# Queries' high parts made by POOL, and the keys' rotation put behind both parts of the queries

## The chip, the cores and the metric

The kernel runs on one core of one Trainium2 chip. The metric is the device time of one execution in microseconds (us). The core's engines run side by side, each with its own list of instructions that it executes in order: TensorE (PE, matmuls), VectorE (DVE), ScalarE (ACT), GpSimd (POOL), and SyncE (SP), which here issues DMA transfers. They meet only at semaphores: an instruction waits until a counter has reached a value that others raise.

## The reference

Rotary attention over 2 batches, 8 heads, 576 tokens and 64 elements per head, then two dense blocks of 512 to 2048 to 512 over all 1152 tokens, the first gated by a sigmoid, the second with an ELU. All in 32-bit floats. Cut to what matters:

```python
def rotate(x):
    x1, x2 = (x[..., :half], x[..., half:])
    return np.concatenate([x1 * cos - x2 * sin, x1 * sin + x2 * cos], axis=-1)
q_rot, k_rot = (rotate(q), rotate(k))
scores = scale * np.matmul(q_rot, k_rot.transpose(0, 1, 3, 2))
scores = scores - np.max(scores, axis=-1, keepdims=True)
attn = np.exp(scores)
attn = attn / (np.sum(attn, axis=-1, keepdims=True) + 1e-09)
x = np.matmul(attn, v)                        # then tokens x 512
h = x @ w_in; x = (h * (1.0 / (1.0 + np.exp(-h)))) @ w_out
h = x @ w_in2; y = np.where(h > 0.0, h, np.exp(np.minimum(h, 0.0)) - 1.0) @ w_out2
```

## The kernel before, in words

**Split numbers.** PE multiplies a rounded 32-bit format (float32r). To keep precision every operand is split into a high part (a copy rounded to float32r) and a low part (the value less its high part), and a product is the sum of three matmuls (high by low, high by high, low by high). So each operand costs a cast and a subtraction on ACT, DVE or POOL.

**Tiles and stages.** The 1152 tokens are three chunks of 384. A chunk has 8 heads, which makes 24 head steps i, each with 3 tiles of 128 queries against 576 keys. A tile goes: scores on PE (L822, L824), negated row maximum on DVE (L620), exponential on ACT (L449), transposes on PE (L838, L847), high part on ACT (L457), low part on DVE (L627). After a head's three tiles come the products with the values (L868, L870) and the steps that scale the output and split it for the dense layers (L475, L651, L657, L482, L662). The dense layers of a chunk are 64 units of weights, 128 x 512 each (L903), each loaded by SP, cast by ACT (L489) and subtracted by POOL (L331). The first chunk's attention runs alone, up to about 65 us (the first stage); the attention of chunks 2 and 3 is spread between the dense units of the chunk before.

**Preparation of queries and keys.** Heads come in pairs, one on partitions 0 to 63 and one on 64 to 127. For pair r the raw queries (`q_raw`, 2 x 384 columns, two buffers) and keys (`k_raw`, 2 x 576 columns, two buffers; only pairs 0 to 7) are loaded. POOL rotates them: two products with the cosine and sine table (L303; keys L286) and their sum (L308; keys L291). ACT casts the high part into the second half of the same buffer (`queries_hi` L434; `keys_hi` L430). POOL subtracts for the low part (`queries_lo` L313; `keys_lo` L296). SP then copies both parts to where PE reads them (`place`, L217 to L223), and after that the buffer is free for the load of pair r + 2. Values are cast by ACT (`values_hi`, L440) and subtracted by POOL (`values_lo`, L318).

**What sets the order.** Nothing is scheduled by a program: each engine's list is written out by hand in loops. In the first stage POOL does, per pair: rotate queries, rotate keys, queries' low part, one weight cast (from the third pair on, L323), keys' low part, values' low part. ACT walks the 24 tiles with `exp_tile(n)` and `probs_hi(n - 1)`, and puts the preparation between them: in the even head of a pair `queries_hi` behind tile 0, `keys_hi` behind tile 1, `values_hi` behind tile 2. Later, in the dense loop, the same steps stand at fixed units j of a head's eight: for example `queries_hi` on ACT at j == 3 of the odd head and `queries_lo` on POOL at j == 5. The queries of pair 5 are rotated just ahead of the dense loop, with their cast on ACT at n == 1.

Of the kernel before, what the change touches and what calls it, by code (L numbers as in the profile page):

```python
# [15 lines left out]
F32R = mybir.dt.float32r  # L16
# [27 lines left out]
def build(nc, q, k, v, rope, w, out):  # L44
    with ExitStack() as ctx:
# [234 lines left out]
        def _(pool):  # L280
# [24 lines left out]
            def queries_add(r):  # L305
                raw = q_raw[r % 2]
                pool.wait_ge(q_scaled, 2 * r)
                nc.gpsimd.tensor_tensor(raw[:, 0, :], raw[:, 0, :], raw[:, 1, :], ALU.add).then_inc(q_roped, 1)  # L308

            def queries_lo(r):  # L310
                raw = q_raw[r % 2]
                pool.wait_ge(q_hi_done, r)
                nc.gpsimd.tensor_tensor(raw[:, 0, :].bitcast(F32R), raw[:, 0, :], raw[:, 1, :], ALU.subtract) \  # L313
                    .then_inc(q_lo_done, 1)
# [33 lines left out]
            def rope_queries(r):  # L348
                queries_times(r, 0)
                queries_times(r, 1)  # L350
                queries_add(r)

            def rope_keys(r):
                keys_times(r, 0)
                keys_times(r, 1)
                keys_add(r)

            rope_queries(1)
            rope_keys(1)
            queries_lo(1)  # L360
            keys_lo(1)
            values_lo(0)
            for p in range(1, 4):
                rope_queries(p + 1)
                rope_keys(p + 1)
                queries_lo(p + 1)
                if p > 1:
                    first_weight_hi(p - 2)
                keys_lo(p + 1)
                values_lo(p)  # L370
            first_weight_hi(2)
            for n in range(AHEAD):
                weight_lo(n)
            rope_queries(5)
            rope_keys(5)
            for n in range(ALL_UNITS):
                i, j = H + n // 8, n % 8
                p = i // 2
                r = p + 2
                if n + AHEAD < ALL_UNITS:  # L380
                    weight_lo(n + AHEAD)
                if n < 2:
                    pool.wait_ge(scored, QN * (7 + n))
                    nc.gpsimd.memset(q_one[n][:, PADS].bitcast(F32), 0.0).then_inc(pads_zero, 1)
                    nc.gpsimd.memset(q_two[n][:, PADS].bitcast(F32), 0.0).then_inc(pads_zero, 1)
                if n == 2:
                    queries_lo(5)
                    keys_lo(5)
                if i % 2 == 0:
                    if j == 5 and p < 8:  # L390
                        values_lo(p)
                    if r < 8:
                        if j == 3:
                            keys_times(r, 0)
                        if j == 4:
                            keys_times(r, 1)
                        if j == 6:
                            keys_add(r)
                    if r < ITERS // 2 and j == 7:
                        queries_times(r, 0)  # L400
                else:
                    if r < ITERS // 2:
                        if j == 0:
                            queries_times(r, 1)
                        if j == 1:
                            queries_add(r)
                    if r < 8 and j == 3:
                        keys_lo(r)
                    if r < ITERS // 2 and j == 5:
                        queries_lo(r)  # L410

# [3 lines left out]
        def _(act):  # L415
# [12 lines left out]
            def keys_hi(r):  # L428
                act.wait_ge(k_roped, r)
                nc.scalar.copy(k_raw[r % 2][:, 1, :].bitcast(F32R), k_raw[r % 2][:, 0, :]).then_inc(k_hi_done, 1)  # L430

            def queries_hi(r):
                act.wait_ge(q_roped, r)
                nc.scalar.copy(q_raw[r % 2][:, 1, :].bitcast(F32R), q_raw[r % 2][:, 0, :]).then_inc(q_hi_done, 1)  # L434

            def values_hi(r):
                act.wait_ge(v_in, 16 * (r + 1))
# [104 lines left out]
            for n in range(H * QN):  # L542
                i, t = n // QN, n % QN
                p = i // 2
                exp_tile(n)
                if n:
                    probs_hi(n - 1)
                if t == 0 and i:
                    end_hi(i - 1)
                if t == 0 and i >= 2:  # L550
                    copy_out_lo(i - 2)
                if i % 2 == 0:
                    if t == 0:
                        queries_hi(p + 1)
                    if t == 1:
                        keys_hi(p + 1)
                    if t == 2:
                        values_hi(p)
                elif p:
                    if t == 0:  # L560
                        widen_sums(p - 1)
                    if t == 2:
                        output_hi(p - 1)
# [3 lines left out]
            for n in range(ALL_UNITS):  # L567
# [21 lines left out]
                    output_hi(p - 1)  # L589
                if not beside:  # L590
                    continue
                if n in (1, 2):
                    (queries_hi if n == 1 else keys_hi)(5)
                if j == 2 and not first:
                    copy_out_lo(i - 1)
                if i % H == H - 1 and j == 7:
# [10 lines left out]
                else:  # L607
                    if j == 0 and p + 2 < 8:
                        keys_hi(p + 2)
                    if j == 3 and p + 2 < ITERS // 2:  # L610
                        queries_hi(p + 2)
            evict_a(ALL_UNITS - 1)


# [436 lines left out]
```

## Time and profile before

| | |
|---|---|
| time, median of 3 runs | 568.55 us (568.23 to 568.56) |
| profiled execution | 568.11 us, its span 566.3 us |
| PE busy | 537.8 us, 95% of the span |
| ACT busy | 349.3 us, 62% |
| POOL busy | 346.8 us, 61% |
| DVE busy | 287.1 us, 51% |

An engine's busy share is a mean over stages that have different limits. The chain that ended last is followed back from the last instruction, at each step to whatever released it; the share of an engine in it says how much of the time that engine's work was what the rest waited for. A timeline row gives the start, the duration, the engine, the line and the tiles, and in brackets how long the engine had been idle before and what ended that. Instructions of one engine can overlap by a few hundredths of a microsecond.

### The profile page before, as it was taken

What the parts mean: (1) busy time and instruction counts of PE and PEld (TensorE: products, weight loads), DVE (VectorE), ACT (ScalarE), POOL (GpSimd) and SP (SyncE); (2) the same over time, 40 slices, a digit from 0 to 9 for tenths busy, and PEclk for the clock granted to TensorE, in tenths of its full rate; (3) what the DMA queues carried; (4) which work ended last, traced back from release to release, by engine and by line L of the source; (5) the groups of instructions that cost most, each with busy time, mean ns of one, the idle gap of its engine ahead of it and who ended that gap; (6) DMA issues with size and microseconds to landing.
All of it is one profiled execution on the core that took longest, in us unless ns stands there. A gap on an engine that the chain in (4) does not pass through costs nothing.

```text
span 566.3 us, 9272 instructions
## 1 busy us (share of the span) xinstructions
PE 537.8 (95%) x3308; PEld 526.8 (93%) x3308; DVE 287.1 (51%) x503; ACT 349.3 (62%) x726; POOL 346.8 (61%) x287
## 2 busy tenths in 40 slices
PE   1888899999999999999999999999999999999997
PEld 1777889999999999999999999989999999999997
DVE  5788766633267763246663336775334540057500
ACT  3899678755467665557785456666555763356531
POOL 5999989669636556555654653444545666655662
PEclk9999999999999999999999999999999999999999
DMA  8676726456355345344333433324433444433440
GB/s 323 186 233 189 218 82 175 114 188 165 97 152 142 90 132 162 106 129 154 116 121 119 128 113 84 105 94 134 120 106 110 132 132 126 131 112 113 131 157 29
DMA packets 43229, 77.16 MB, mean 136 GB/s; under 512 B 5296, under 2 KB 12848, under 8 KB 43184
## 3 DMA queue, kind: packets, MB, share of 16 engines
q1 hardware_dynamic: 41456, 74.21, 44.4%
q10 hardware_dynamic: 1728, 2.36, 1.1%
q8 instruction: 27, 0.44, 0.3%
q14 instruction: 18, 0.15, 0.1%
HBM read 63.57 MB, written 2.36 MB: 116 GB/s over the span
## 4 chain that ended last, share of the span: by engine, by line
PE 79%; DVE 10%; ACT 6%; issue 3%; DMA 1%; SPq 0%; ACTq 0%; DVEq 0%
PE banks L903 61%; PE banks L868 5%; PE banks L838 5%; PE banks L822 3%; PE banks L824 3%; DVE banks L692 2%; DVE act_buf L690 2%; ACT prob L449 2%; DVE neg_max L620 2%; ACT act_buf L501 1%; PE banks L847 1%; DVE pt_lo L627 1%; DMA k_raw<-k 1%; DVE g_lo L698 1%; ACT g_hi L508 1%
## 5 line engine op out<-in xcount | busy, mean ns | idle before, releaser
L331 POOL TENSOR_TENSOR w_lo<-w_raw,w_hi 128x512 fp32r<-128x512 f32 x192 | 247.0, 1288 | 201.4 <-ACT w_hi L489 201.0
L489 ACT CAST w_hi<-w_raw 128x512 fp32r<-128x512 f32 x189 | 117.1, 621 | 40.3 <-PE banks L903 36.1
L903 PE MATMUL banks<-x_lo,w_hi 128*128 128x384 f32 x384 | 130.7, 340 | 1.5 <-DVE g_lo L698 0.8
L903 PE MATMUL banks<-g_lo,w_hi 128*128 128x384 f32 x384 | 129.1, 336 | 0.0
L903 PE MATMUL banks<-x_hi,w_lo 128*128 128x384 f32 x384 | 128.7, 335 | 0.0
L903 PE MATMUL banks<-x_hi,w_hi 128*128 128x384 f32 x384 | 128.6, 335 | 0.0
L903 PE MATMUL banks<-g_hi,w_lo 128*128 128x384 f32 x384 | 128.5, 335 | 0.0
L903 PE MATMUL banks<-g_hi,w_hi 128*128 128x384 f32 x384 | 128.5, 335 | 0.0
L627 DVE TENSOR_TENSOR pt_lo<-banks,pt_hi 128x512 fp32r<-128x512 f32 x60 | 41.3, 688 | 93.5 <-ACT pt_hi L457 93.4
L449 ACT ACTIVATE prob<-banks,neg_max 128x576 f32<-128x576 f32 x72 | 53.6, 744 | 42.5 <-DVE neg_max L620 42.2
L903 PEld LDWEIGHTS banks<-x_lo,w_hi 128*128 128x128 f32 x384 | 72.1, 188 | 5.0 <-DVE x_lo L662 1.6
L698 DVE SCALAR_TENSOR_TENSOR g_lo<-banks,g_hi 128x384 fp32r<-128x384 f32 x96 | 53.4, 556 | 40.5 <-ACT g_hi L508 40.2
L903 PEld LDWEIGHTS banks<-g_lo,w_hi 128*128 128x128 f32 x384 | 72.1, 188 | 0.1
L903 PEld LDWEIGHTS banks<-x_hi,w_hi 128*128 128x128 f32 x384 | 72.2, 188 | 0.0
L903 PEld LDWEIGHTS banks<-g_hi,w_hi 128*128 128x128 f32 x384 | 72.2, 188 | 0.0
L903 PEld LDWEIGHTS banks<-g_hi,w_lo 128*128 128x128 f32 x384 | 72.1, 188 | 0.0
L903 PEld LDWEIGHTS banks<-x_hi,w_lo 128*128 128x128 f32 x384 | 72.1, 188 | 0.0
L508 ACT ACTIVATE g_hi<-banks 128x384 fp32r<-128x384 f32 x96 | 47.4, 493 | 35.6 <-DVE banks L692 30.6
L822 PE MATMUL banks<-k_st,q_one 128*128 128x288 f32 x160 | 51.8, 340 | 11.5 <-DVE q_two L676 11.4
L501 ACT ACTIVATE act_buf<-banks 128x384 f32<-128x384 f32 x96 | 46.9, 489 | 21.1 <-PE banks L903 21.0
L620 DVE TENSOR_REDUCE neg_max<-banks 128x1 f32<-128x576 f32 x72 | 54.0, 750 | 6.6 <-PE banks L824 6.0
L838 PE MATMUL banks<-ident,prob 128*128 128x128 f32 x288 | 44.9, 279 | 10.9 <-ACT prob L449 10.5
(75 smaller groups left out, 696.0 us busy)
## 6 DMA issues: line engine op xcount, KB each, us to landing
w_raw<-w SPq DMA_DIRECT2D x192, 256.0 KB, 2.7
q_raw<-q SPq DMA_DIRECT2D x11, 384.0 KB, 3.5
q_one<-q_raw SPq DMA_DIRECT2D x44, 96.0 KB, 2.5
k_raw<-k SPq DMA_DIRECT2D x7, 576.0 KB, 4.5
k_st<-k_raw SPq DMA_DIRECT2D x28, 144.0 KB, 2.5
v_raw<-v SPq DMA_DIRECT2D x8, 320.0 KB, 3.1
out<-act_buf ACTq DMA_DIRECT2D x12, 192.0 KB, 2.7
q_two<-q_raw SPq DMA_DIRECT2D x22, 96.0 KB, 2.3
```

Source lines behind the costliest of these rows:

```text
L331: nc.gpsimd.tensor_tensor(w_st[LO][:, slot, :], w_raw[:, slot, :], w_st[HI][:, slot, :].bitcast(F32), ALU.subtract).then_inc(w_lo_done, 1)
L449: nc.scalar.activation(halves(prob[:, n % 3, :]), scores(n), ACT.Exp, bias=neg_max[:, n % 2:n % 2 + 1], accum_out=row_sum[:, i // 2 % 2, t ...
L489: nc.scalar.copy(w_st[HI][:, slot, :], w_raw[:, slot, :]).then_inc(w_hi_done, 1)
L501: nc.scalar.activation(act_buf[:, ft % 2, :], mlp(USES * c + 20 * layer + ft), func, scale=scale) \
L508: nc.scalar.activation(g[HI][:, ft, :], mlp(USES * c + 20 * layer + ft), ACT.Copy, scale=(0.5, 1.0)[layer]).then_inc(g_hi_done, 1)
L620: nc.vector.tensor_reduce(neg_max[:, n % 2:n % 2 + 1], scores(n), AXES.XY, ALU.max, negate=True) \
L627: nc.vector.tensor_tensor(pt[LO][buffer_of(i)][:, :, tokens], probs_t(n), pt[HI][buffer_of(i)][:, :, tokens].bitcast(F32), ALU.subtract) \
L698: nc.vector.scalar_tensor_tensor(g[LO][:, ft, :], mlp(USES * c + 20 * layer + ft), (0.5, 1.0)[layer], g[HI][:, ft, :].bitcast(F32), ALU.mu ...
L822: nc.tensor.matmul(scores(n)[:, a, :], q_one[par][:, col:col + P], k_st[:, slot, keys], start=m == 0, stop=False)
L838: last = nc.tensor.transpose(probs_t(n)[:, m, :], prob[:, n % 3, m * P:(m + 1) * P], ident[:, :])
L868: nc.tensor.matmul(pv_out[:, cols], v_st[:, slot, m, :], pt[part][buf][:, m, cols], start=m == 0 and part == LO, stop=False)
L903: last = nc.tensor.matmul(dst, w_st[wp][:, slot, m * P:(m + 1) * P], src[xp][:, tile, :], start=start and n == 0, stop=stop and n == 2)
```

## The change

POOL gets a function `queries_hi`, which copies the queries' sum, rounded, into the second half of the buffer, and ACT loses its function of that name with its 11 calls. In the first stage POOL's order per pair becomes: rotate queries, high part, low part, then rotate keys, and so on; for pair 5 the high part stands ahead of the keys' rotation and the low part stays where it was; for later pairs the high part is made at j == 4 of the odd head. Nothing else differs. (Line numbers behind the edit move: L313 of the new kernel is the new cast, and its `queries_lo` is L318.)

```diff
--- before.py
+++ after.py
@@ -307,6 +307,11 @@
                 pool.wait_ge(q_scaled, 2 * r)
                 nc.gpsimd.tensor_tensor(raw[:, 0, :], raw[:, 0, :], raw[:, 1, :], ALU.add).then_inc(q_roped, 1)
 
+            def queries_hi(r):
+                raw = q_raw[r % 2]
+                pool.wait_ge(q_roped, r)
+                nc.gpsimd.tensor_copy(raw[:, 1, :].bitcast(F32R), raw[:, 0, :]).then_inc(q_hi_done, 1)
+
             def queries_lo(r):
                 raw = q_raw[r % 2]
                 pool.wait_ge(q_hi_done, r)
@@ -356,14 +361,16 @@
                 keys_add(r)
 
             rope_queries(1)
+            queries_hi(1)
+            queries_lo(1)
             rope_keys(1)
-            queries_lo(1)
             keys_lo(1)
             values_lo(0)
             for p in range(1, 4):
                 rope_queries(p + 1)
+                queries_hi(p + 1)
+                queries_lo(p + 1)
                 rope_keys(p + 1)
-                queries_lo(p + 1)
                 if p > 1:
                     first_weight_hi(p - 2)
                 keys_lo(p + 1)
@@ -372,6 +379,7 @@
             for n in range(AHEAD):
                 weight_lo(n)
             rope_queries(5)
+            queries_hi(5)
             rope_keys(5)
             for n in range(ALL_UNITS):
                 i, j = H + n // 8, n % 8
@@ -406,6 +414,8 @@
                             queries_add(r)
                     if r < 8 and j == 3:
                         keys_lo(r)
+                    if r < ITERS // 2 and j == 4:
+                        queries_hi(r)
                     if r < ITERS // 2 and j == 5:
                         queries_lo(r)
 
@@ -428,10 +438,6 @@
             def keys_hi(r):
                 act.wait_ge(k_roped, r)
                 nc.scalar.copy(k_raw[r % 2][:, 1, :].bitcast(F32R), k_raw[r % 2][:, 0, :]).then_inc(k_hi_done, 1)
-
-            def queries_hi(r):
-                act.wait_ge(q_roped, r)
-                nc.scalar.copy(q_raw[r % 2][:, 1, :].bitcast(F32R), q_raw[r % 2][:, 0, :]).then_inc(q_hi_done, 1)
 
             def values_hi(r):
                 act.wait_ge(v_in, 16 * (r + 1))
@@ -550,8 +556,6 @@
                 if t == 0 and i >= 2:
                     copy_out_lo(i - 2)
                 if i % 2 == 0:
-                    if t == 0:
-                        queries_hi(p + 1)
                     if t == 1:
                         keys_hi(p + 1)
                     if t == 2:
@@ -589,8 +593,8 @@
                     output_hi(p - 1)
                 if not beside:
                     continue
-                if n in (1, 2):
-                    (queries_hi if n == 1 else keys_hi)(5)
+                if n == 2:
+                    keys_hi(5)
                 if j == 2 and not first:
                     copy_out_lo(i - 1)
                 if i % H == H - 1 and j == 7:
@@ -607,8 +611,6 @@
                 else:
                     if j == 0 and p + 2 < 8:
                         keys_hi(p + 2)
-                    if j == 3 and p + 2 < ITERS // 2:
-                        queries_hi(p + 2)
             evict_a(ALL_UNITS - 1)
```

POOL's list in the first stage, one pair (the one whose queries are rotated from 20.78 us on). Before; `q_raw` and `k_raw` are the raw and rotated queries and keys, `v_st` the values, and in brackets stand the semaphores waited for:

```order
L303 TENSOR_TENSOR q_raw<-q_raw,table 128x384 [waits q_in0]
L303 TENSOR_TENSOR q_raw<-q_raw,table 128x384
L308 TENSOR_TENSOR q_raw<-q_raw 128x384 [waits q_scaled]
L286 TENSOR_TENSOR k_raw<-k_raw,k_table 128x576 [waits k_table_in,k_in0]
L286 TENSOR_TENSOR k_raw<-k_raw,k_table 128x576
L291 TENSOR_TENSOR k_raw<-k_raw 128x576 [waits k_scaled]
L313 TENSOR_TENSOR q_raw<-q_raw 128x384 [waits q_hi_done]
L296 TENSOR_TENSOR k_raw<-k_raw 128x576 [waits k_hi_done]
L318 TENSOR_TENSOR v_st<-v_raw,v_st 128x2x5x64 [waits v_hi_done]
```

The same pair in the changed kernel:

```order
L303 TENSOR_TENSOR q_raw<-q_raw,table 128x384 [waits q_in0]
L303 TENSOR_TENSOR q_raw<-q_raw,table 128x384
L308 TENSOR_TENSOR q_raw<-q_raw 128x384 [waits q_scaled]
L313 CAST q_raw<-q_raw 128x384 [waits q_roped]
L318 TENSOR_TENSOR q_raw<-q_raw 128x384 [waits q_hi_done]
L286 TENSOR_TENSOR k_raw<-k_raw,k_table 128x576 [waits k_table_in,k_in0]
L286 TENSOR_TENSOR k_raw<-k_raw,k_table 128x576
L291 TENSOR_TENSOR k_raw<-k_raw 128x576 [waits k_scaled]
L296 TENSOR_TENSOR k_raw<-k_raw 128x576 [waits k_hi_done]
L323 TENSOR_TENSOR v_st<-v_raw,v_st 128x2x5x64 [waits v_hi_done]
```

The sum of the keys (L291) stood behind five instructions of its pair and stands behind seven; between it and the keys' low part (L296), which waits for ACT's cast of the keys, stood the queries' low part, and now nothing does.

ACT's list for the same pair, before; `prob` is an exponential's tile, `pt_hi` the transposed one's high part:

```order
L475 COPY head_out<-banks 64x384 [waits pv_done]
L434 CAST q_raw<-q_raw 128x384 [waits q_roped]
L449 ACTIVATE prob,row_sum<-banks,neg_max 128x576 [waits end_transposed,max_done]
L457 CAST pt_hi<-banks 128x4x128 [waits pv_done,transposed]
L430 CAST k_raw<-k_raw 128x576 [waits k_roped]
L449 ACTIVATE prob,row_sum<-banks,neg_max 128x576 [waits end_transposed,max_done]
L457 CAST pt_hi<-banks 128x4x128 [waits transposed]
L440 CAST v_st<-v_raw 128x2x5x64 [waits v_in]
```

And in the changed kernel:

```order
L481 COPY head_out<-banks 64x384 [waits pv_done]
L455 ACTIVATE prob,row_sum<-banks,neg_max 128x576 [waits end_transposed,max_done]
L463 CAST pt_hi<-banks 128x4x128 [waits pv_done,transposed]
L440 CAST k_raw<-k_raw 128x576 [waits k_roped]
L455 ACTIVATE prob,row_sum<-banks,neg_max 128x576 [waits end_transposed,max_done]
L463 CAST pt_hi<-banks 128x4x128 [waits transposed]
L446 CAST v_st<-v_raw 128x2x5x64 [waits v_in]
```

The cast of `q_raw` is gone; the cast of `k_raw`, which waits for the keys' sum (`k_roped`), stands where it stood, with the same instructions behind it.

## Rows read from the trace of the kernel before

**Rows 1.** from the page: busy us by engine, and the chain by engine

```profile
PE 537.8 (95%) x3308; PEld 526.8 (93%) x3308; DVE 287.1 (51%) x503; ACT 349.3 (62%) x726; POOL 346.8 (61%) x287
...
PE 79%; DVE 10%; ACT 6%; issue 3%; DMA 1%; SPq 0%; ACTq 0%; DVEq 0%
```

**Rows 2.** windows: stretch, length, busy us (instructions) by engine, PEclk, DMA share, GB/s

```profile
14.00:62.00 48.00, 39.18 (x269) 36.30 (x270) 40.29 (x68) 43.87 (x99) 44.37 (x38) 1.00 0.70 194
82.00:92.00 10.00, 10.00 (x62) 9.96 (x61) 7.52 (x14) 8.55 (x19) 10.00 (x9) 1.00 0.52 153
```

**Rows 3.** timeline of ACT: start, duration, instruction, idle before

```profile
16.55 0.67 ACT L430 CAST k_raw<-k_raw 128x576 fp32r<-128x576 f32 x1 [0.45 <-POOL k_raw L291]
...
28.45 0.68 ACT L430 CAST k_raw<-k_raw 128x576 fp32r<-128x576 f32 x1
...
30.21 0.75 ACT L440 CAST v_st<-v_raw 128x640 fp32r<-128x640 f32 x1
...
41.48 0.68 ACT L430 CAST k_raw<-k_raw 128x576 fp32r<-128x576 f32 x1
...
54.52 0.68 ACT L430 CAST k_raw<-k_raw 128x576 fp32r<-128x576 f32 x1
...
61.56 0.74 ACT L449 ACTIVATE prob<-banks,neg_max 128x576 f32<-128x576 f32 x1 [0.54 <-DVE neg_max L620]
...
74.61 0.51 ACT L434 CAST q_raw<-q_raw 128x384 fp32r<-128x384 f32 x1
```

**Rows 4.** timeline of POOL, 9 to 63 us

```profile
9.25 1.95 POOL L303 TENSOR_TENSOR q_raw<-q_raw,table 128x384 f32<-128x384 f32 x2 [0.50 <-DVE banks L730]
...
15.10 1.41 POOL L291 TENSOR_TENSOR k_raw<-k_raw 128x576 f32<-128x576 f32 x1
...
19.27 1.54 POOL L318 TENSOR_TENSOR v_st<-v_raw,v_st 128x640 fp32r<-128x640 f32 x1 [0.43 <-ACT v_st L440]
20.78 1.96 POOL L303 TENSOR_TENSOR q_raw<-q_raw,table 128x384 f32<-128x384 f32 x2
22.81 1.01 POOL L308 TENSOR_TENSOR q_raw<-q_raw 128x384 f32<-128x384 f32 x1
23.78 2.81 POOL L286 TENSOR_TENSOR k_raw<-k_raw,k_table 128x576 f32<-128x576 f32 x2
26.67 1.41 POOL L291 TENSOR_TENSOR k_raw<-k_raw 128x576 f32<-128x576 f32 x1
...
32.55 1.96 POOL L303 TENSOR_TENSOR q_raw<-q_raw,table 128x384 f32<-128x384 f32 x2
...
45.59 1.96 POOL L303 TENSOR_TENSOR q_raw<-q_raw,table 128x384 f32<-128x384 f32 x2
...
51.47 1.63 POOL L291 TENSOR_TENSOR k_raw<-k_raw 128x576 f32<-128x576 f32 x1
...
59.18 3.74 POOL L331 TENSOR_TENSOR w_lo<-w_raw,w_hi 128x512 fp32r<-128x512 f32 x3
```

**Rows 5.** groups by form, POOL: count, busy us, mean ns, idle before

```profile
L313 POOL TENSOR_TENSOR q_raw<-q_raw 128x384 fp32r<-128x384 f32 x11 | 11.1, 1008 | 0.5 <-ACT q_raw L434 0.5
...
L323 POOL CAST w_hi<-w_raw 128x512 fp32r<-128x512 f32 x3 | 1.8, 612 | 0.0
```

**Rows 6.** timeline of PE, waits at the end of the stage

```profile
60.60 0.33 PE L838 MATMUL banks<-ident,prob 128*128 128x128 f32 x1 [1.37 <-ACT prob L449]
...
64.73 0.34 PE L903 MATMUL banks<-x_lo,w_hi 128*128 128x384 f32 x1
...
72.27 0.44 PE L903 MATMUL banks<-x_lo,w_hi 128*128 128x384 f32 x1 [0.74 <-DVE x_lo L662]
...
80.36 0.66 PE L838 MATMUL banks<-ident,prob 128*128 128x128 f32 x4 [0.51 <-ACT prob L449]
```

**Rows 7.** timeline of PE, matmuls of 288 columns

```profile
17.33 0.44 PE L824 MATMUL banks<-k_st,q_two 128*128 128x288 f32 x1
...
18.93 0.29 PE L822 MATMUL banks<-k_st,q_one 128*128 128x288 f32 x1
```

## The prediction

> **What bounds the kernel now.** I read the page's chain first [rows 1]: TensorE (PE) carries 79% of it, ScalarE (ACT) 6% and VectorE (DVE) 10%, and POOL none of its listed lines. So the changed instructions are not on the bound by themselves, and the question is where they gate something. The windows [rows 2] split the program into two regimes. In 82 to 92 us, inside the dense layers, PE is busy 10.00 of 10.00 us; what another engine does there is hidden as long as its slots suffice. In 14 to 62 us, the attention of the first eight heads, no engine is full, but ACT (43.87 of 48 us) and POOL (44.37 of 48 us) come close and PE does not (39.18). That stage is set by engines handing work to each other, and the order of instructions on ACT and POOL is what counts. It works in four pairs of heads (I number them 1 to 4; the pair's preparation is for the next heads).
>
> The timeline of ACT [rows 3] has, in each pair, the cast of the queries' high parts (L434, 0.51 us as the one at 74.61, which stands in the dense layer), then an exponential, a copy, and the cast of the keys' high parts (L430). L430 needs the keys' sum from POOL (L291). POOL's timeline [rows 4] gives when that sum is there. Pair 1: sum ends 15.10 + 1.41 = 16.51, L430 starts 16.55 after a wait of 0.45. Pair 2: 26.67 + 1.41 = 28.08 against 28.45, slack 0.37. Pair 4: 51.47 + 1.63 = 53.10 against 54.52, slack 1.42. Pair 3 repeats pair 4 to 0.01 us, 13.04 us earlier (L430 at 41.48), so its sum ends 40.06. That slack is the number the change works on.
>
> **What is removed.** ACT loses 11 casts of 0.51 us. Four stand in the first stage, one (74.61) [rows 3] early in the first dense layer, six later, where PE is full.
>
> **What is added and moved on POOL.** In each of the four pairs the keys' rotation now stands behind two instructions more: the high cast and the low subtraction. The trace has no 384-element cast on POOL; the nearest row is its 512-element cast at 0.612 us [rows 5]. Bounds: 0.46 us (scaled by elements) and 0.61 us (none of it scales). I take 0.50, near the scaled end, because the subtractions show a small fixed part: 1.008 us for 384 elements [rows 5], 1.25 us from start to start for 512 (59.18, three in 3.74) [rows 4]. The sum of the queries starts 22.81 and lasts 1.01; before, the keys started at 23.78. Now: 22.81 + 1.01 + 0.07 (the gap that POOL shows before an instruction that waits for its predecessor, 20.78 + 1.96 to 22.81) + 0.50 + 0.07 + 0.96 (the subtraction of 1.008 less the 0.05 that consecutive starts overlap) = 25.42, so **1.64 us later** per pair; by the bounds 1.60 to 1.75.
>
> The Trainium skill (GPSIMD Engine Reference, section 3.1) gives as best case of a tight one-input loop 1.8 cycles per element, 769 ns for 512 elements. This trace has 612 ns for 512, so the measurement decides; by the page the 384-element cast would be an estimated 576 ns and the sum below 0.3 us longer.
>
> **What that meets.** ACT executes in order. Behind the waiting L430 stand the next exponential, the copy of the transposed tile and the cast of the values (L440), for which POOL's last step of the pair (L318) waits. So POOL and ACT form a loop: pair start S, keys' sum end, 0.04, ACT's run from L430 to the end of L440 (28.45 to 30.21 + 0.75 = 2.51), 0.07, values' low part 1.51 start to start (19.27 to 20.78), next S. The old low subtraction and the weight cast used to stand between sum and keys' low part; that cover goes, and POOL idles while ACT casts the keys. Walking it:
> - Pair 1: S = 9.25. Sum end 16.51 + 1.64 = 18.15, L430 at 18.19 (was 16.55), next S = 18.19 + 4.09 = 22.28 (was 20.78).
> - Pair 2: before, S to sum end took 28.08 - 20.78 = 7.30; now 8.94. L430 at 31.26 (was 28.45), next S 35.35 (was 32.55).
> - Pair 3: 7.51 as in pair 4, now 9.15. L430 at 35.35 + 9.15 + 0.04 = 44.54 (was 41.48), next S 48.63 (was 45.59).
> - Pair 4: 53.10 - 45.59 = 7.51, now 9.15. L430 at 57.82 (was 54.52): **+3.30 us**.
>
> So the first two pairs lose 1.6 and 1.2 and the others 0.25 each, since there POOL had been waiting for ACT and the 0.51 us that ACT saves just turns into a longer wait at L430. Does ACT really arrive early? It reaches L430 of pair 4 no later than 54.52 + 3.06 (the lateness in pair 3) - 0.51 = 57.1, before 57.82. Yes, and likewise in pair 3.
>
> **What is given back.** After the last L430 ACT runs without a gap until the exponential at 61.56, which waited 0.54 for a maximum of DVE [rows 3]. PE and DVE have run on during ACT's hold, so I take 0.46 of that back: the dense layer, whose first matmul stood at 64.73 [rows 6], starts 2.84 later. POOL must have the first three weights' low parts by then: they began 59.18 and took 3.74 [rows 4], now 3.3 later, ending 66.2 against 67.6: covered, though the margin shrinks from 1.8 to 1.4. In 70 to 82 us the chain passes L434 at 74.61; without it the activation behind it starts some 0.4 earlier, and the PE wait of 0.51 at 80.36 [rows 6] shrinks by that much. After that PE is full and nothing is regained; the six POOL casts of the later pairs (6 x 0.50) lie in POOL's idle time (it is busy 61% of the span [rows 1]), and ACT's six saved casts lie beside PE. On SP the query placements of each pair now start earlier, the key placements later by the same shift as ACT; I count nothing for them.
>
> Sum: 3.30 - 0.46 - 0.40 = +2.44 us. The profiled execution took 568.11 (span 566.3 and 1.8 around it), so it would take 570.55; the median of the runs is 568.55, 0.44 above it, so I predict **571.0 us**. With the bounds of the cast (-0.04 x 4, +0.11 x 4), 0 to 0.54 given back at the exponential and 0 to 0.5 at L434, the likeliest case spans 570.7 to 572.3.
>
> **Rivals.**
> 1. *The slack absorbs it.* The most the tail can give back is what PE waited there: 1.37 at 60.60, 0.74 at 72.27, 0.51 at 80.36 [rows 6], together 2.62. Then 3.30 - 2.62 = +0.7, about 569.25. For it: DVE and PE had finished their part during the hold. Against: the first and second of these waits are for ACT's and DVE's steps that themselves shift. Chance 0.14.
> 2. *Faster: ACT's relief wins.* If the keys' sum still came before ACT asked for it, five casts of 0.51 on the chain would go: 2.5 us, 566.0. It decides only if the delay on POOL stays below the slack of the pair: 1.64 against 0, 0.37 and twice 1.42. That holds only if most of the inserted 1.5 us runs under something. For it: L434 is on the chain of waits in pairs 2 to 4 and is surely removed. Against: POOL shows no idle place before the sum. Chance 0.08.
> 3. *The array's clock.* The page's granted clock is 1.00 throughout, yet the matmuls of 288 columns take 0.44 us at 17.33 and 0.29 at 18.93 [rows 7], the pace of the 1.2 and of the 2.4 GHz level, so PE came up near 18 us after steady work. A hold of ACT would leave PE idle some 1.6 us per pair, more than the 1.37 us at 60.60, after which the dense matmul at 64.73 still took 0.34 us. If the clock fell in pairs 2 to 4: a pair holds 39.18 x 13.04 / 48 = 10.6 us of PE [rows 2], 0.44 / 0.29 = 1.5 times as long at the slow pace, thus 5.3 us more; for half of the pair 2.7, less some 0.9 by which ACT is early at the next hold: 3 x 1.8 = 5.4, about 576.4. Chance 0.06. The Trainium skill (TensorE: Matmul & The Clock Gate, section "HAM oscillation") says that pauses between bursts can bring the slow clock back each time; this trace shows no fall after the pause of 1.37 us.
>
> **How the numbers follow.** Forecast 0.72, rivals 0.14, 0.08 and 0.06. A measurement of this kernel tells about 0.2%, 1.1 us, from no change. Slower by more than that: 0.72 + 0.06 = 0.78; within: 0.14; faster: 0.08. Range for 8 in 10: from 569.4, near the first rival, to 572.5, just over the likeliest case's end.
>
> **What would show it.** In the new profile: the 11 L434 casts gone from ACT and 11 POOL casts of about 0.50; keys' high casts at about 18.2, 31.3, 44.5 and 57.8 with waits of 1 to 2 us on POOL's sum; POOL waiting about 0.7 for them; the first dense matmul near 67.6; from 85 us on the same work shifted by about 2.4. It is wrong if ACT does not wait at the keys' cast, if the POOL cast takes well under 0.4 us, or if PE's wait near 82 vanishes with more than 0.5.

## The result, and the profile after

| | before | after |
|---|---|---|
| time, median of 6 runs | 568.55 us (568.17 to 568.70) | 572.46 us (571.21 to 572.77) |
| ratio | | 1.0066 (95% interval 1.0053 to 1.0079) |
| profiled execution | 568.11 us, span 566.3 | 572.77 us, span 570.7 |

The change makes the kernel slower by 0.66%, 3.9 us between the medians. That is forecast in sign and inside the range, but 1.5 us above the predicted 571.0.

From the page after: PE's share of the busy time, the granted clock in 40 slices, and the chain by engine, which now has POOL in it [rows 1].

```profile
PE 541.9 (95%) x3308; PEld 530.5 (93%) x3308; DVE 288.6 (51%) x503; ACT 345.1 (60%) x715; POOL 352.6 (62%) x298
...
PEclk9989999999999999999999999999999999999999
...
PE 78%; DVE 9%; ACT 6%; issue 4%; POOL 2%; DMA 1%; SPq 0%; ACTq 0%; DVEq 0%; POOLq 0%
```

POOL's timeline after, first pair (start, duration, instruction, idle before). The cast takes 0.50 us; the sum of the keys starts at 16.75 instead of 15.10 [rows 4], and then POOL idles 0.78 us for ACT's cast of the keys.

```profile
12.36 0.50 POOL L313 CAST q_raw<-q_raw 128x384 fp32r<-128x384 f32 x1
12.94 1.00 POOL L318 TENSOR_TENSOR q_raw<-q_raw 128x384 fp32r<-128x384 f32 x1
13.90 2.77 POOL L286 TENSOR_TENSOR k_raw<-k_raw,k_table 128x576 f32<-128x576 f32 x2
16.75 1.42 POOL L291 TENSOR_TENSOR k_raw<-k_raw 128x576 f32<-128x576 f32 x1
18.95 1.41 POOL L296 TENSOR_TENSOR k_raw<-k_raw 128x576 fp32r<-128x576 f32 x1 [0.78 <-ACT k_raw L440]
```

ACT's timeline after: the four casts of the keys (L430 before, L440 now). Three wait for POOL's sum, the third does not.

```profile
18.20 0.67 ACT L440 CAST k_raw<-k_raw 128x576 fp32r<-128x576 f32 x1 [2.09 <-POOL k_raw L291]
...
31.29 0.67 ACT L440 CAST k_raw<-k_raw 128x576 fp32r<-128x576 f32 x1 [1.12 <-POOL k_raw L291]
...
45.18 0.68 ACT L440 CAST k_raw<-k_raw 128x576 fp32r<-128x576 f32 x1
...
59.21 0.67 ACT L440 CAST k_raw<-k_raw 128x576 fp32r<-128x576 f32 x1 [0.70 <-POOL k_raw L291]
```

Before, they stood at 16.55, 28.45, 41.48 and 54.52 [rows 3]. The first two are where the prediction put them (18.19, 31.26). The last two are late by 0.6 and 1.4 us more, and PE's timeline shows where most of that comes from (experiment 1 gives its size): after an idle of 1.55 us its matmuls of 288 columns take 0.44 us, the pace of the 1.2 GHz level [rows 7], until about 41 us.

```profile
37.33 1.00 PE L840 MATMUL banks<-ident,prob 128*128 128x128 f32 x4 [1.55 <-ACT prob L455]
...
38.36 0.44 PE L826 MATMUL banks<-k_st,q_two 128*128 128x288 f32 x1
...
41.09 0.29 PE L826 MATMUL banks<-k_st,q_two 128*128 128x288 f32 x1
```

The windows after give the granted clock there (the column behind POOL's): 0.94, then 0.64. The kernel before has 1.00 in both.

```profile
34.00:38.00 4.00, 1.91 (x14) 1.63 (x13) 3.51 (x6) 3.93 (x10) 3.92 (x4) 0.94 0.56 135
38.00:42.00 4.00, 4.00 (x23) 3.98 (x22) 2.09 (x4) 1.92 (x5) 3.86 (x5) 0.64 0.76 193
```

### The profile page after: what moved, and what is told of

It reads as the page before. It is cut to its first block, busy times and chain, and to the rows that moved or that the text cites. A ratio compares the mean times of both kernels' runs of the same rounds, so it can differ in the third digit from the quotient of the medians.

```text
span 570.7 us, 9272 instructions
## 1 busy us (share of the span) xinstructions
PE 541.9 (95%) x3308; PEld 530.5 (93%) x3308; DVE 288.6 (51%) x503; ACT 345.1 (60%) x715; POOL 352.6 (62%) x298
## 4 chain that ended last, share of the span: by engine, by line
PE 78%; DVE 9%; ACT 6%; issue 4%; POOL 2%; DMA 1%; SPq 0%; ACTq 0%; DVEq 0%; POOLq 0%
PE banks L905 62%; PE banks L870 4%; PE banks L840 4%; PE banks L824 3%; PE banks L826 3%; DVE banks L694 2%; ACT prob L455 2%; DVE act_buf L692 2%; DVE neg_max L622 2%; ACT act_buf L507 1%; PE banks L849 1%; DMA k_raw<-k 1%; DVE pt_lo L629 1%; ACT g_hi L514 1%; PE banks L883 1%
## 5 line engine op out<-in xcount | busy, mean ns | idle before, releaser
L336 POOL TENSOR_TENSOR w_lo<-w_raw,w_hi 128x512 fp32r<-128x512 f32 x192 | 247.4, 1290 | 197.6 <-ACT w_hi L495 197.2
L824 PE MATMUL banks<-k_st,q_one 128*128 128x288 f32 x160 | 53.1, 347 | 11.4 <-DVE q_two L678 11.4
L840 PE MATMUL banks<-ident,prob 128*128 128x128 f32 x288 | 46.7, 287 | 11.1 <-ACT prob L455 10.9
```

The costliest lines, as they stand in the source:

```text
L336: nc.gpsimd.tensor_tensor(w_st[LO][:, slot, :], w_raw[:, slot, :], w_st[HI][:, slot, :].bitcast(F32), ALU.subtract).then_inc(w_lo_done, 1)
L824: nc.tensor.matmul(scores(n)[:, a, :], q_one[par][:, col:col + P], k_st[:, slot, keys], start=m == 0, stop=False)
L840: last = nc.tensor.transpose(probs_t(n)[:, m, :], prob[:, n % 3, m * P:(m + 1) * P], ident[:, :])
```

## The experiments

Each kernel was timed against the kernel before on the same chip; the medians of before there were 568.20 to 568.27.

**1. The changed kernel again** (no edit).

> The changed kernel once more, unaltered, for a second profile and more times. The first profile showed matmuls of 288 columns at 0.44 us between 37 and 40 us and a granted clock of 0.87 there; two of its six runs took 571.2 to 571.5 at a mean clock of 0.999, four took 572.4 to 572.8 at 0.997. Theory A (the keys' late sum holds ACT, and the clock adds a part of its own): the runs fall in these two groups again, 571.3 with a mean clock of 0.999 and 572.5 with 0.997, and the base of the loss is the lower one. Theory B (the clock's fall is only a symptom): times do not sort by the mean clock.

Measured: 571.68 us median of 5 runs (571.53 to 573.15), ratio 1.0066 (1.0054 to 1.0078). Over the 11 runs of both series, five took 571.2 to 571.7 (median 571.5) at mean clocks of 0.997 to 1.0, six took 572.4 to 573.2 (median 572.6) at 0.994 to 0.997. So there are two groups, 1.1 us apart, but the mean clock does not sort them strictly: the profiled execution, 571.59 us, has 0.997. Its windows show where its slow stretch lies, which is ahead of 26 us:

```profile
18.00:22.00 4.00, 2.27 (x15) 1.76 (x15) 2.37 (x4) 3.61 (x8) 2.79 (x3) 0.96 0.37 89
22.00:26.00 4.00, 4.00 (x23) 3.85 (x22) 3.22 (x5) 3.19 (x8) 3.86 (x5) 0.61 0.44 102
```

It cost nothing there, because POOL sets the pace: the first two casts of the keys stand 13.10 us apart, against 31.29 - 18.20 = 13.09 in the first profile, where the clock was 1.00 in that stretch. Where the clock falls matters, not only whether. In the first profile it fell in 34 to 42 us, and from POOL's first step to ACT's fourth cast of the keys that execution takes 59.21 - 9.26 = 49.95 us, this one 58.26 - 9.47 = 48.79: 1.16 more, the distance between the groups. This trace is the clean case, and I use it for the balance below. ACT's casts of the keys in it, each waiting for POOL:

```profile
18.39 0.67 ACT L440 CAST k_raw<-k_raw 128x576 fp32r<-128x576 f32 x1 [2.08 <-POOL k_raw L291]
...
31.49 0.67 ACT L440 CAST k_raw<-k_raw 128x576 fp32r<-128x576 f32 x1 [1.30 <-POOL k_raw L291]
...
44.88 0.67 ACT L440 CAST k_raw<-k_raw 128x576 fp32r<-128x576 f32 x1 [0.69 <-POOL k_raw L291]
...
58.26 0.68 ACT L440 CAST k_raw<-k_raw 128x576 fp32r<-128x576 f32 x1 [0.69 <-POOL k_raw L291]
```

**2. The low part back behind the keys** (in the changed kernel).

```diff
             queries_hi(1)
-            queries_lo(1)
             rope_keys(1)
+            queries_lo(1)
```

(and the same in the loop over the pairs)

> POOL keeps the cast right behind the queries' sum, but the low part goes back behind the keys' rotation in the first stage. The keys' sum is then late by 0.57 us per pair instead of 1.64. Theory A (what costs is how late the keys' sum is when ACT asks for it): S to sum 7.83, 7.87, 8.08, 8.08; keys' casts at about 17.1, 29.1, 41.5 and 54.0; 568.0 (567.4 to 568.8), no slower than the kernel before. Theory B (the 0.5 us more of POOL's work per pair is what costs, wherever it stands): about the same as the changed kernel, 571 to 572.

Measured: 569.54 us (569.34 to 570.84), ratio 1.0028 (1.0017 to 1.0039). Two thirds of the loss go with this move, though POOL does the same work: place decides, not amount. It stays 1.3 us above before, where I expected none. The casts of the keys are at 17.28, 29.26, 42.54 and 55.52. The first two wait for the sum (1.00 and 0.42 us) and stand near the expected 17.1 and 29.1. The last two, expected at 41.5 and 54.0, wait for nothing: there ACT itself is late, behind a wait of 1.26 us at 38.35 for DVE's scaled output, and PE had before that waited 0.46 us for a placement of the keys at 36.41. So the sum's lateness is not the whole of this kernel's loss. It also carries the collision of experiments 7 and 8 (DVE's step takes 1.03 us here).

**3. Both parts behind the keys** (in the changed kernel).

```diff
-            queries_hi(1)
-            queries_lo(1)
             rope_keys(1)
+            queries_hi(1)
+            queries_lo(1)
```

> In the first stage POOL makes the queries' high and low parts behind the keys' rotation, so that they cover ACT's cast of the keys. The keys' sum is not late at all within the pair, ACT keeps its 0.51 us per pair. Theory A: no wait of ACT at the keys' casts in pairs 2 to 4, POOL's period is 11.8 to 12.6 us against ACT's 12.5; the dense layer starts 1.0 to 1.4 us earlier than in the kernel before; 567.0 (566.3 to 567.8), faster than before. Theory B (POOL's work itself costs): 570 to 572.

Measured: 568.86 us (567.51 to 570.71, 12 runs), ratio 1.0010 (0.9999 to 1.0021): no change, and a spread of 3 us. The loss of the change is gone with POOL's extra work still in place, but the gain that I expected did not come. The casts of the keys are at 16.79, 28.86, 41.91 and 54.58, unhindered; but POOL ends the pair later, the placements follow, and PE now waits for one:

```profile
23.51 0.37 PE L824 MATMUL banks<-k_st,q_one 128*128 128x288 f32 x1 [0.74 <-DMA k_st<-k_raw]
```

Six of the twelve runs lie at 567.5 to 568.4 and six at 569.3 to 570.7. Four of the slower six have a mean clock of 1.0, so the clock does not make this split; its cause stays open.

**4. One more cast on POOL in each pair of the changed kernel.**

```diff
                 pool.wait_ge(q_roped, r)
+                if r < 5:
+                    nc.gpsimd.tensor_copy(spare[:, :], raw[:, 0, 0:352])
                 nc.gpsimd.tensor_copy(raw[:, 1, :].bitcast(F32R), raw[:, 0, :]).then_inc(q_hi_done, 1)
```

> The changed kernel, with one more cast of 352 columns into an unused tile ahead of the queries' cast for pairs 1 to 4 (its result is not used). It makes the keys' sum another 0.42 to 0.47 us late in each pair. Theory A: since POOL sets the period, each of the four pairs adds the whole 0.45, thus 1.8 us: 573.0 in a run without the slow clock, 574.3 with it. Theory of slack (the loss is a step of the first two pairs, later ones absorb it): at most 0.9 us more.

Measured: 573.46 us (572.67 to 574.21, 4 runs), ratio 1.0090 (1.0077 to 1.0103). From POOL's first step of the queries to ACT's fourth cast of the keys the trace of experiment 1 has 58.26 - 9.47 = 48.79 us and this one 59.22 - 8.71 = 50.51: 1.72 more, 0.43 in each of four pairs. Nothing is absorbed. (The first steps differ by 0.76 because the first transfers landed earlier in this execution.)

**5. Extra transposes behind PE's wait** (eight in front of tiles 10, 16 and 22).

```diff
+                for _ in range(8 if n in (10, 16, 22) else 0):
+                    nc.tensor.transpose(probs_t(n)[:, 0, :], ident[:, :], ident[:, :])
                 for m in range(4):
```

> The changed kernel, with eight extra transposes of the identity on PE ahead of the transposes of tiles 10, 16 and 22, into the bank that those overwrite; PE idles there for 1.55 us in the profile in which the matmuls ran at half pace from 37 to 41 us. Theory A (part of the loss is the clock falling after that pause): the granted clock is 1.00 from 30 us on in the profile, the group of slower runs (572.4 to 573.2) goes, all runs lie at 571.3 to 571.8. A fall near 20 us may stay, since nothing is filled there and it cost nothing in the second profile. Theory B (the slower group has another cause): the spread stays, 571.5 to 573, or the extra work makes all runs slower by up to 2.6 us.

Measured: 574.15 us (573.82 to 577.75), ratio 1.0116 (1.0097 to 1.0136). The edit was misplaced: the transposes stood behind the wait for the exponential, so the idle stayed 1.55 us and they were added to the path, 3 x 0.9 = 2.7. It does not test what it was made for. It does show that the clock can cost more than 1.1 us: four runs have a mean clock of 0.999 or 1.0 (573.82 to 574.25, median 574.0), two have less (575.51 at 0.997, 577.75 at 0.994). The last is the profiled one, with the clock down in two stretches (0.66 in 38 to 42 us, 0.75 in 66 to 70 us), 3.75 us above that median. The kernel serves as the base of experiment 7.

**6. The same transposes ahead of that wait.**

```diff
+                if n in (10, 16, 22):
+                    pe.wait_ge(pt_lo_done, n - 1)
+                    for _ in range(8):
+                        nc.tensor.transpose(probs_t(n)[:, 0, :], ident[:, :], ident[:, :])
                 pe.wait_ge(exp_done, n + 1)
```

> The changed kernel, with the eight extra transposes of the identity ahead of PE's wait for the exponential of tiles 10, 16 and 22 (in the kernel named filler they stood behind that wait, on the path, and cost 0.9 us each). They wait only for what the bank's overwriting waits for and fill 0.9 of the 1.55 us that PE idles. Theory A (the slower group of runs comes from the clock falling after that pause): no slow matmuls behind 30 us, all runs 571.3 to 571.9. Theory B: the runs at 572.4 to 573.2 stay, with falls of the clock at other places or none.

Measured: 571.55 us (571.38 to 571.80, 5 runs), ratio 1.0059 (1.0047 to 1.0071), clock 0.999 or 1.0 in each run. PE's timeline and the windows of this kernel: the idle is cut to 0.44, the clock stays.

```profile
35.59 1.09 PE L835 MATMUL banks<-ident 128*128 128x128 f32 x8
37.12 0.66 PE L844 MATMUL banks<-ident,prob 128*128 128x128 f32 x4 [0.44 <-ACT prob L455]
```

```profile
34.00:38.00 4.00, 3.15 (x23) 2.69 (x24) 3.52 (x6) 3.93 (x10) 3.92 (x4) 1.00 0.56 131
38.00:42.00 4.00, 4.00 (x32) 3.97 (x31) 3.38 (x6) 3.17 (x9) 3.86 (x5) 1.00 0.73 187
```

More work on PE, and the slower group (6 of 11 runs) is gone in 5 of 5. If it were still there at the old rate, five runs without it would come up in (5/11)^5, 2 of 100 cases. The chip is not the reason: experiments 9 and 10 ran on the same one and have runs at a mean clock of 0.996 or 0.997. With the two profiles of experiment 1 this says that the slower group is the clock falling after such an idle, for 1.1 to 1.2 us. Five runs are few, though: two of the five faster runs of the changed kernel have a mean clock of 0.997, one of them with the fall ahead of 26 us, and that early fall is missing here too, where nothing was filled. Of the six slower runs one has a trace. In it the idle of 1.55 us comes three times (at 37.33, 51.84 and 65.24), and the clock fell after the first alone; in the clean trace it comes three times as well (at 37.52, 50.91 and 64.29), with no fall after any.

**7. The transposes of experiment 5, and POOL waits for DVE.** The kernel named filler is the base.

```diff
+                if n == 0:
+                    pool.wait_ge(x_lo_done, 4)
                 if n + AHEAD < ALL_UNITS:
                     weight_lo(n + AHEAD)
```

> As the kernel with the extra transposes, and POOL's weight subtraction for unit 3 waits until DVE has made the fourth low part of the dense layer's input (1.04 us beside that subtraction, 0.56 without, in the profiles). Theory A (the late POOL now runs beside that step of DVE and slows it): the step takes 0.56, PE's wait ahead of the dense layer's last tile of the first unit falls by 0.48, and the time by 0.3 to 0.5 us against the kernel with the extra transposes. Theory B (DVE's step is long for another reason, or PE's wait has another end): no change, or slower because the weights come later.

Measured: 573.60 us (573.46 to 573.80), ratio 1.0094 (1.0081 to 1.0107); 0.55 below experiment 5, and 0.40 below its four runs whose clock did not fall; it fell in none of these. The wait for DVE is what differs, but the trace of experiment 5 cannot show the collision that it removes: in that one execution, in which the clock fell twice, DVE's step stands at 81.78 with no subtraction beside it and takes 0.56 us. Experiment 8 is the clearer test. What is meant is seen in the trace of experiment 1, all engines around 75 us: POOL's subtraction (L336) overlaps DVE's low part of the dense input (L664), which takes 1.03, and PE waits 1.20 for it.

```profile
74.68 1.29 POOL L336 TENSOR_TENSOR w_lo<-w_raw,w_hi 128x512 fp32r<-128x512 f32 x1
...
75.34 1.03 DVE L664 TENSOR_TENSOR x_lo<-head_out,x_hi 128x384 fp32r<-128x384 f32 x1 [0.58 <-ACT x_hi L488]
...
76.43 0.44 PE L905 MATMUL banks<-x_lo,w_hi 128*128 128x384 f32 x1 [1.20 <-DVE x_lo L664]
```

In the kernel before, POOL had just ended (70.41 + 1.28 = 71.69) when DVE began at 71.65; DVE took 0.56 and PE waited 0.74 [rows 6]:

```profile
70.41 1.28 POOL L331 TENSOR_TENSOR w_lo<-w_raw,w_hi 128x512 fp32r<-128x512 f32 x1
...
71.65 0.56 DVE L662 TENSOR_TENSOR x_lo<-head_out,x_hi 128x384 fp32r<-128x384 f32 x1 [0.58 <-ACT x_hi L482]
```

**8. The change in the dense part only**, without and with that wait (dense_only and dense_port). The edit is the diff of the change without its lines for the first stage; the second kernel has the two lines of experiment 7 as well.

> The kernel before, with the change made only for the queries of pairs 5 and later: ACT keeps its casts and POOL its order in the first stage. Theory A: nothing of the loss of 3.3 us lies here; ACT's cast early in the dense layer goes (0.33 back in the changed kernel), but the cast of pair 5 on POOL makes the weight subtraction 0.57 later, so that it meets DVE's step (0.48 lost): 568.4 (567.9 to 568.8), no change. Theory B (POOL's casts in the dense layers cost, as its other work there is on the path): slower by 0.5 us or more per cast, 570 or above.

> The change for pairs 5 and later only, and POOL's weight subtraction for unit 3 waits for DVE's step. Theory A: DVE's step at 0.56 us as in the kernel before, ACT's cast gone: 567.9 (567.4 to 568.3), 0.3 to 0.5 below the same kernel without the wait. Theory B: the wait changes nothing.

Measured: 568.36 us (567.46 to 568.52, 11 runs), ratio 0.9998 (0.9989 to 1.0007), and 567.50 us (567.04 to 567.85, 11 runs), ratio 0.9985 (0.9977 to 0.9994). So on balance the dense part costs nothing, and moving POOL out of DVE's way is worth 0.86 between these medians, of which the two traces show 0.50 (DVE's step takes 1.06 us without the wait and 0.56 with it). The second kernel is the only one here that is faster than before by more than its interval, by 0.15%. Its trace, DVE's step undisturbed:

```profile
71.63 0.56 DVE L670 TENSOR_TENSOR x_lo<-head_out,x_hi 128x384 fp32r<-128x384 f32 x1 [0.58 <-ACT x_hi L492]
...
72.27 1.28 POOL L336 TENSOR_TENSOR w_lo<-w_raw,w_hi 128x512 fp32r<-128x512 f32 x1 [1.24 <-DVE x_lo L670]
```

It also shows a second gain. In the kernel before, an ACT cast of the queries late in chunk 2's attention was on the path: DVE waited 0.78 us for the activation behind it, then came DVE's later steps up to its low part, and PE's next unit after a gap of 201.03 - 200.31 = 0.72.

```profile
194.91 0.50 ACT L434 CAST q_raw<-q_raw 128x384 fp32r<-128x384 f32 x1
...
195.84 0.55 DVE L690 SCALAR_TENSOR_TENSOR act_buf<-act_buf,banks 128x384 f32<-128x384 f32 x1 [0.78 <-ACT act_buf L501]
...
200.31 0.34 PE L903 MATMUL banks<-x_hi,w_lo 128*128 128x384 f32 x1
...
200.34 0.55 DVE L698 SCALAR_TENSOR_TENSOR g_lo<-banks,g_hi 128x384 fp32r<-128x384 f32 x1
...
201.03 0.41 PE L903 MATMUL banks<-x_lo,w_hi 128*128 128x384 f32 x1 [0.39 <-DVE g_lo L698]
```

Without it (dense_port) DVE's wait is 0.36 and the gap 0.31:

```profile
195.10 0.56 DVE L698 SCALAR_TENSOR_TENSOR act_buf<-act_buf,banks 128x384 f32<-128x384 f32 x1 [0.36 <-ACT act_buf L511]
...
199.60 0.55 DVE L706 SCALAR_TENSOR_TENSOR g_lo<-banks,g_hi 128x384 fp32r<-128x384 f32 x1
...
199.99 0.34 PE L911 MATMUL banks<-x_hi,w_lo 128*128 128x384 f32 x1
...
200.30 0.41 PE L911 MATMUL banks<-x_lo,w_hi 128*128 128x384 f32 x1
```

**9. Both parts behind the keys, high part of one column** (edit: the kernel of experiment 3 with `cols = slice(0, 1 if r < 5 else CT)` in the cast).

> The kernel with both parts behind the keys' rotation, but in the first stage the queries' high part is copied for one column of 384 only, the rest of it is left out. POOL does 0.4 us less per pair, ACT's cast is gone as well. Theory A (in that kernel the POOL work of the pair and the later placements took what ACT's missing cast would have given): placements 0.4 us earlier, no wait of PE for them, 567.3 (566.6 to 568.0). Theory B (ACT's cast in the first stage was worth nothing, since DVE and PE set the period): as the kernel with both parts behind, 568.3 or above.

Measured: 568.06 us (567.10 to 570.45, 12 runs), ratio 1.0003 (0.9991 to 1.0016). The one-column cast takes 0.19 us, so POOL does 0.3 us less per pair and not 0.4. Undecided: the seven faster runs (567.1 to 568.2) lie near what theory A asks, five others at 569.2 to 570.5. The profiled one (569.77) has both a wait of 0.88 us for a placement at 36.06 and a granted clock of 0.70 in 38 to 42 us. What ACT's missing casts are worth in the first stage stays open.

**10. Both parts behind the keys, and POOL waits for DVE** (the edits of experiments 3 and 7).

> Both parts of the queries behind the keys' rotation in the first stage, and POOL's weight subtraction for unit 3 waits for DVE's step. Theory A: 0.5 us below the kernel without that wait: 568.2 (567.0 to 569.0), with the same spread of 2 us or more, which comes from PE waiting for late placements. It would have to reach 567.0 to beat the kernel with the change in the dense part alone. Theory B: no change.

Measured: 567.05 us (566.58 to 570.34, 12 runs), ratio 0.9992 (0.9980 to 1.0005). Seven runs at 566.6 to 567.2, five at 568.4 to 570.3. The median is 1.8 below experiment 3, where I expected 0.5, but both kernels have two groups and the median jumps between them; between the medians of the faster groups (566.87 and 567.79) it is 0.9. Its best runs are the fastest of all, but its interval takes in no change, so the kernel with the change in the dense part and the wait is the better-proven version.

**11. The order alone**, ACT keeping its casts.

```diff
             rope_queries(1)
+            queries_lo(1)
             rope_keys(1)
-            queries_lo(1)
```

(on the kernel before, and the same in the loop)

> The order alone: ACT keeps making the queries' high parts, but POOL in the first stage makes the low part ahead of the keys' rotation, so it waits for ACT's cast before it can go on to the keys. Theory A (POOL and ACT form a loop, and what counts is how late the keys' sum is): keys' casts at about 20.1, 36, 52 and 68 us, a period near 16 us; the dense layer starts 13 us later, 581 (579 to 584), with the array's clock falling in the longer pauses of PE. Theory B (each engine catches up in its slack, the loss of the change is its POOL work): below 574.

Measured: 585.29 us (584.69 to 585.89, 4 runs), ratio 1.0300 (1.0287 to 1.0314). POOL's timeline: the low part waits for ACT, 2.50 and then 4.22 us, and the keys stand behind it.

```profile
14.93 1.00 POOL L313 TENSOR_TENSOR q_raw<-q_raw 128x384 fp32r<-128x384 f32 x1 [2.50 <-ACT q_raw L434]
...
31.54 0.99 POOL L313 TENSOR_TENSOR q_raw<-q_raw 128x384 fp32r<-128x384 f32 x1 [4.22 <-ACT q_raw L434]
```

ACT in turn waits at the keys' casts, which stand at 20.18, 36.80, 53.96 and 71.14. The first two fit (20.1, 36). The period is 17.2 instead of 16: from a cast of the keys to the next cast of the queries ACT takes 48.11 - 36.80 = 11.31 us, as much as in the kernel before (52.78 - 41.48 = 11.30), and from there it is 53.96 - 48.11 = 5.85 to the next cast of the keys. The loop is what it was said to be; the time is 4 us above what I expected, and outside the range. With ACT's casts the new order costs 17 us, with POOL's it costs 3.3 when the clock holds. The clock fell in all four runs (0.985 in the mean; 0.58 in 38 to 42 us in the trace), and how much of the 17 us it takes is not separated.

## Why the prediction was right, and where its size was off

**Right, and shown.** The inserted 1.64 us is 16.75 - 15.10 = 1.65, the cast 0.50. ACT is held at the keys' casts, POOL idles 0.78 for them, and the loss accumulates per pair (experiments 2, 3, 4 and 11 make the keys' sum less late, not late, later and much later, and the time follows, in experiment 2 only in part through this wait). From POOL's first step to the fourth cast of the keys: predicted +3.30, in the clean trace (58.26 - 9.47) - (54.52 - 9.25) = +3.52. ACT's waits at the four casts, 2.08, 1.30, 0.69 and 0.69, are the pattern of the walk. The missing 0.2 lies in pairs 3 and 4: the keys' two products (L286) now run beside DVE's low part of the dense input and take 3.12 us instead of 2.80, while their sum, which met that step before, takes 1.41 instead of 1.63. The walk had moved the old durations along.

**Sizes off, in the clean case.** The balance of spans, 569.6 - 566.3 = +3.3, against the predicted +2.44:

| term | predicted | measured | from |
|---|---|---|---|
| POOL's first step later (transfers, not the change) | 0 | +0.22 | 9.47 against 9.25 |
| fourth cast of the keys | +3.30 | +3.52 | ACT's rows |
| given back at the exponential and behind | -0.46 | -0.05 | last output's cast at 74.80 against 71.11 |
| POOL beside DVE at the dense input | 0 | +0.47 | PE resumes at 76.43 against 72.27 |
| ACT's cast for pair 5 gone | -0.40 | -0.35 | PE's wait of 0.51 at 80.36 is 0.16 |
| a later cast of ACT gone | 0 | -0.4 | ACT's rows stand 3.80 later until 188 us, 3.40 later from 195 us on |
| not assigned | 0 | -0.1 | rest of the sum |

The give-back failed as a step, but not where I had put it. The wait of 0.54 at the exponential did go: that instruction stands 64.70 - 61.56 = 3.14 later, the ones ahead of it 3.69 (63.41 against 59.72). Two instructions on, ACT waits 0.64 for DVE's scaled output, and everything is 3.69 late again. In the kernel before:

```profile
62.37 0.56 DVE L657 TENSOR_TENSOR head_out<-head_out,banks 128x384 f32<-128x384 f32 x1
...
62.96 0.51 ACT L482 CAST x_hi<-head_out 128x384 fp32r<-128x384 f32 x1
```

In the clean trace of the changed kernel:

```profile
64.70 0.74 ACT L455 ACTIVATE prob<-banks,neg_max 128x576 f32<-128x576 f32 x1
...
66.06 0.56 DVE L659 TENSOR_TENSOR head_out<-head_out,banks 128x384 f32<-128x384 f32 x1 [0.62 <-PE banks L883]
...
66.65 0.51 ACT L488 CAST x_hi<-head_out 128x384 fp32r<-128x384 f32 x1 [0.64 <-DVE head_out L659]
```

That chain starts at the exponential ahead of the one that waited and goes through PE's transposes (64.29 against 60.60, also 3.69 later) to DVE's output step. The wait of 0.54 was not on it. So the first dense matmul stands at 68.43, not near 67.6. The prediction counted the casts of the later pairs at nothing "beside PE"; one of them was worth 0.4 (experiment 8). And it checked only that POOL's first three weight parts came in time, not what its fourth would now run beside: that is the +0.47, shown in experiments 7 and 8.

**The clock.** The prediction carried it as a rival, with 0.06 and 5.4 us, and as the other case to the forecast. It is no rival but an addition: by the two groups it happened in 6 of 11 runs, on top of the mechanism forecast, for 1.1 us (experiments 1 and 6), since it fell once and came back within 4 us. Its chance was far too low. Its price of 5.4 took three falls of 1.8 each; one fall in the traced execution cost 1.16. The median of the first series, 572.46, is one of runs with the fall. That it lies inside the range, 0.04 below its end, is luck, since that end was not meant for the clock. The faster group, at 571.5, is what the forecast of 571.0 was about. It came so near because errors partly cancel: the give-back and the collision cost 0.9 more than forecast, and the later cast of ACT gave 0.4 back. The argument against it, that the dense matmuls after a pause of 1.37 us were fast, was weak: one pause in one execution. The first rival (the tail absorbs it) and the second (ACT's relief wins) are refuted by the casts' times. Even with the keys' sum not late (experiment 3), the relief did not show as time.

## What to carry to other kernels

Before a step is put ahead of another on an engine with slack, ask which engine will ask for the result of the other, and what that engine has queued behind its wait: here a step of 0.50 us and one of 1.0 us moved ahead of the keys' rotation (with 0.5 us saved on ACT in each pair) cost 3.3 us, since two in-order engines waited for each other once per pair. Then ask what a late engine will run beside, since a step that has time to spare can still slow another engine's. A kernel whose matmuls stand behind a repeated idle can lose the clock in some of its runs, here in 6 of 11; look at the clock by windows in more than one profile.

## What the runs showed of the hardware that I had not expected

- DVE's subtraction of 128x384 with all operands in SBUF takes 0.56 us alone, and the first unit's takes 1.00 to 1.06 beside a POOL subtraction (in seven kernels); keeping POOL away by a wait gained 0.40 (at equal clocks) and 0.86 us of kernel time in two comparisons. When it starts at least 0.1 us into a single two-input step of POOL, with at least 0.1 us of that left, it ends 0.40 to 0.42 us after that step's end, whether it began 0.14 us into it (1.85 us long, at 134.14 in the clean trace) or 0.66 (1.03 us, at 75.34). When DVE's step starts first, POOL's is the one that takes longer: in the trace of experiment 3 DVE's at 38.86 keeps its 0.55 us and POOL's sum of the keys, begun at 38.87, takes 1.82 instead of 1.41. The Trainium skill (GPSIMD Engine Reference, section "Key points") says that POOL shares its SBUF interfaces with VectorE and contends with instructions that have two SBUF inputs; the traces agree.
- The array's clock fell in one traced execution after one of three idles of 1.55 us and in another of the same kernel after none of them, and the mean clock was 0.999 or 1.0 in all five runs when 1.1 us of each was filled. The Trainium skill (TensorE: Matmul & The Clock Gate, section "HAM oscillation — how this bites in real kernels") describes kernels whose clock falls between bursts of matmuls; the profiled execution with the fall agrees (0.64 in 38 to 42 us after that idle).
